# Layer norm's statistics moved within the layer, weight pieces worked two steps later, and the second MLP's tokens loaded one layer earlier, in a three-stage kernel

## The reference

```
kv = k^T v per head;  out = q kv;  out = out / rms(out) * g_norm
x  = out as (batch, token, 512)
u  = x + real(fft2(x));  un = layernorm(u)
x2 = u + relu(un @ w_ch1) @ w_ch2            (512 -> 2048 -> 512)
u2 = x2 + (x2^T @ U @ V)^T                   (tokens mixed, rank 32)
out = u2 + relu(u2 @ w2_ch1) @ w2_ch2
```

## Time and profile before

| | |
|---|---|
| median of 3 runs | 1805.35 us (1803.37 to 1811.79) |
| the profiled execution: its own time | 1805.91 us |
| its span, first to last instruction | 1804.1 us |
| granted TensorE clock, mean | 0.985 of full speed |
| busy share of the span: PE, DVE, ACT, POOL | 95%, 77%, 44%, 20% |
| DMA: moved, mean | 478.53 MB, 265 GB/s |

### The profile page before, as it was taken

One profiled execution on the slowest core, in us unless ns is written; L12 is line 12 of the kernel. 1 busy time (PEld: TensorE's weight loads), 2 busy tenths in 40 slices (PEclk: granted clock), 3 DMA queues, 4 the chain that ended last, 5 costly groups with the idle time before them and its releaser, 6 DMA issues.

```text
span 1804.1 us, 27550 instructions
## 1 busy us (share of the span) xinstructions
PE 1721.0 (95%) x10772; PEld 1659.3 (92%) x10772; DVE 1381.1 (77%) x1679; ACT 784.9 (44%) x1126; POOL 364.4 (20%) x308
## 2 busy tenths in 40 slices
PE   6789979989999999999999999999999999999999
PEld 5667769979998999999999999999999999999999
DVE  4779986997797788887876866956947757758567
ACT  2333334644554554554444445435434434443443
POOL 2889974231010010010010021010100100100200
PEclk9899989999999999999999999999999999999999
DMA  7477557998788798898887777866766756767663
GB/s 259 152 269 248 198 199 273 338 346 323 285 331 305 288 342 304 298 344 305 310 311 240 251 251 256 320 231 238 252 234 246 266 210 252 252 222 260 230 243 128
DMA packets 124977, 478.53 MB, mean 265 GB/s; under 512 B 12401, under 2 KB 49777, under 8 KB 84146
## 3 DMA queue, kind: packets, MB, share of 16 engines
q1 hardware_dynamic: 123634, 475.60, 74.3%
q10 hardware_dynamic: 1216, 1.18, 0.2%
HBM read 398.09 MB, written 78.64 MB: 264 GB/s over the span
## 4 chain that ended last, share of the span: by engine, by line
PE 75%; DVE 14%; DMA 3%; issue 3%; POOL 3%; ACT 1%; SPq 1%; DVEq 0%; POOLq 0%; ACTq 0%
PE pair L869 11%; PE pair L871 10%; PE pair L870 10%; PE pair L900 6%; PE pair L901 6%; PE pair L902 6%; PE pair L889 5%; PE pair L892 5%; PE pair L891 5%; DVE t_lo L1406 3%; PE pair L672 2%; DMA in_sb<-x_dram 1%; DVE t_raw L1425 1%; PE tr_ps L765 1%; DVE w_sb L1338 1%
## 5 line engine op out<-in xcount | busy, mean ns | idle before, releaser
L869 PE MATMUL pair<-t_hi,w_sb 128*128 128x384 f32 x1344 | 459.9, 342 | 10.1 <-DVE h_sb L1443 8.3
L870 PE MATMUL pair<-t_lo,w_sb 128*128 128x384 f32 x1344 | 455.7, 339 | 0.0
L871 PE MATMUL pair<-t_hi,w_sb 128*128 128x384 f32 x1344 | 455.6, 339 | 0.0
L1643 POOL TENSOR_TENSOR t_raw<-a_sb 128x768 f32<-128x768 f32 x60 | 127.2, 2124 | 1206.9 <-PE pair L892 476.1
L1116 ACT ACTIVATE t_hi<-t_raw 128x768 fp32r<-128x768 f32 x240 | 202.6, 847 | 278.9 <-DVE t_raw L1425 278.9
L1406 DVE TENSOR_TENSOR t_lo<-t_raw,t_hi 128x768 fp32r<-128x768 f32 x300 | 306.4, 1026 | 9.5 <-ACT t_hi L1104 8.2
L889 PE MATMUL pair<-w_sb,t_hi 128*128 128x256 f32 x1008 | 285.4, 283 | 8.0 <-DVE t_lo L1406 8.0
L891 PE MATMUL pair<-w_sb,t_hi 128*128 128x256 f32 x1008 | 283.5, 281 | 0.0
L892 PE MATMUL pair<-w_sb,t_lo 128*128 128x256 f32 x1008 | 283.5, 281 | 0.0
L869 PEld LDWEIGHTS pair<-t_hi,w_sb 128*128 128x128 f32 x1344 | 252.6, 188 | 17.6 <-issue 12.4
L870 PEld LDWEIGHTS pair<-t_lo,w_sb 128*128 128x128 f32 x1344 | 252.8, 188 | 3.0
(11 more groups left out here) (158 smaller groups left out, 2370.5 us busy)
## 6 DMA issues: line engine op xcount, KB each, us to landing
w_sb<-wc SPq DMA_DIRECT2D x268, 1024.0 KB, 5.2
wc<-w_sb SPq DMA_DIRECT2D x20, 1024.0 KB, 6.5
w_raw<-wr1a SPq DMA_DIRECT2D x24, 512.0 KB, 5.7
w_raw<-wr1b SPq DMA_DIRECT2D x24, 512.0 KB, 4.1
wc<-pb SPq DMA_DIRECT2D x16, 640.0 KB, 4.8
w_raw<-wr2a SPq DMA_DIRECT2D x10, 1024.0 KB, 7.3
wc<-pb_v SPq DMA_DIRECT2D x16, 640.0 KB, 5.4
q_sb<-q_t SPq DMA_DIRECT2D x8, 1152.0 KB, 9.3
```

The lines of the kernel that those rows point to most:

```text
L869: nc.tensor.matmul(ps, w_hi, hi[:, x, :], start=(fresh and x == 0), stop=False, skip_group_check=True)
L870: nc.tensor.matmul(ps, w_hi, lo[:, x, :], start=False, stop=False, skip_group_check=True)
L871: last = nc.tensor.matmul(ps, w_lo, hi[:, x, :], start=False, stop=(x == 1), skip_group_check=True)
```

## The change

`LN_AT` goes from 14, 17, 26 to 8, 13, 26, so statistics stand at 8, 13, 26 and the normalising at 10, 15, 28. `load_in` at steps 2 and 4 stays for the layers up to 6; the first four chunks of layers 7 to 11 (normed or mixed, and turned, one layer before the products use them) are asked for at steps 44 and 46 of the layer before that, g = 5 to 9, instead of steps 2 and 4 of g = 6 to 10. Unit and job: the sum from t+4 to t+6, ACT's split from t+7 to t+8, DVE's from t+8 to t+9, the store from t+8 to t+10.

```diff
--- before.py
+++ after.py
@@ -149,7 +149,7 @@
 
 OUT_AT = [1 + 3 * j for j in range(NCH)]
 GATHER_AT = [4 + 3 * j for j in range(NCH)]
-LN_AT = [14, 17, 26]
+LN_AT = [8, 13, 26]
 
 
 def mix_at(g):
@@ -633,21 +633,25 @@
                         store_u(B - 1)
 
                     if g < NG - 1:
-                        if t in (2, 4):
+                        if t in (2, 4) and g + 1 <= NS:
                             load_in(NCH * (g + 1) + t - 2)
                             load_in(NCH * (g + 1) + t - 1)
+
+                        if t in (44, 46) and NS < g + 2 < NG:
+                            load_in(NCH * (g + 2) + t - 44)
+                            load_in(NCH * (g + 2) + t - 43)
                         if t in in_load_at(g):
                             load_in(NCH * (g + 1) + 4 + in_load_at(g).index(t))
 
                     if (g, t) in UNIT_AT:
                         load_unit(UNIT_AT[g, t])
-                    if (g, t - 8) in UNIT_AT:
-                        store_unit(UNIT_AT[g, t - 8])
+                    if (g, t - 10) in UNIT_AT:
+                        store_unit(UNIT_AT[g, t - 10])
 
                     if (g, t) in JOB_AT:
                         load_job(JOB_AT[g, t])
-                    if (g, t - 8) in JOB_AT:
-                        store_job(JOB_AT[g, t - 8])
+                    if (g, t - 10) in JOB_AT:
+                        store_job(JOB_AT[g, t - 10])
                     n = NSLOT * g + j
                     if n + 3 in RAW_SLOTS and stored_slot(n + 3):
                         store_w(n + 3)
@@ -1229,10 +1233,10 @@
                             take_in(NCH * (g + 1) + in_at(g).index(t - 1))
                         if g + 1 < NS and t - 1 in LN_AT:
                             deviation(3 * (g + 1) + LN_AT.index(t - 1))
-                    if (g, t - 7) in UNIT_AT:
-                        split_unit_hi(UNIT_AT[g, t - 7])
-                    if (g, t - 7) in JOB_AT:
-                        split_job_hi(JOB_AT[g, t - 7])
+                    if (g, t - 8) in UNIT_AT:
+                        split_unit_hi(UNIT_AT[g, t - 8])
+                    if (g, t - 8) in JOB_AT:
+                        split_job_hi(JOB_AT[g, t - 8])
                     for n in RAW_SLOTS:
                         if NSTEP * g + t == max(0, 2 * n - 7):
                             split_slot_hi(n)
@@ -1577,14 +1581,14 @@
                                 layer_norm(3 * (g + 1) + LN_AT.index(t - 2))
                         elif t - 1 in mix_at(g):
                             add_mixed(NCH * (g + 1) + mix_at(g).index(t - 1))
-                    if (g, t - 4) in UNIT_AT:
-                        sum_unit(UNIT_AT[g, t - 4])
-                    if (g, t - 4) in JOB_AT:
-                        sum_job(JOB_AT[g, t - 4])
-                    if (g, t - 8) in UNIT_AT:
-                        split_unit_lo(UNIT_AT[g, t - 8])
-                    if (g, t - 8) in JOB_AT:
-                        split_job_lo(JOB_AT[g, t - 8])
+                    if (g, t - 6) in UNIT_AT:
+                        sum_unit(UNIT_AT[g, t - 6])
+                    if (g, t - 6) in JOB_AT:
+                        sum_job(JOB_AT[g, t - 6])
+                    if (g, t - 9) in UNIT_AT:
+                        split_unit_lo(UNIT_AT[g, t - 9])
+                    if (g, t - 9) in JOB_AT:
+                        split_job_lo(JOB_AT[g, t - 9])
                     for n in RAW_SLOTS:
                         if NSTEP * g + t == max(0, 2 * n - 6):
                             split_slot_lo(n)
```

## The result

The changed kernel takes 1797.4 us (median of 10 runs, 1792.65 to 1801.31) against 1806.3 us (10 runs, 1801.99 to 1812.91): a ratio of 0.995, 95% interval 0.9931 to 0.9969. The forecast was 1795.2 us. The profiled execution has a span of 1796.1 us against 1804.1, 8.0 us less. Every ratio in this document is against executions of the kernel before that were taken alongside, and leaves out three slow ones: 1826.2 us of the kernel before (experiments 1 to 4), and 2359.5 and 2110.9 us of the 11 in experiment 6.

The account below looks back on a forecast made before the run. PE, busy 1721.0 of 1804.1 us, was taken to bound the kernel, its waits all ending with late DVE results. The sum was 1805.91 - 18.1 (parts 1 and 2) + 7.2 + 0.2 = 1795.2 us, range 1786.5 to 1804.5.

Parts of the forecast that it names:

- Part 1, tokens a layer ahead: Layers 7 to 10: PE's waits on the first mixed chunk vanish, gain 7.6 us; layer 7's own move brings nothing.
- Part 2, what leaves steps 6, 14 and 17: Waits after step 7 (4.4 us) and at step 19 (5.3 us in layers 1 to 4, 0.8 in layer 0) vanish.
- Part 3, what comes late: Layers 1 to 4: new PE waits at four places, 1.8 us a layer, 7.2 in four; layer 0 loses 0.2.
- step 13: Layers 1 to 4: `x_lo` for the gather after this step late by 0.6 us, its slot's low part held by POOL.
- step 16: Layers 1 to 4: gather late by 0.5 us, as step 15's normalising stands before m7 and `x_lo`.
- step 24: Layers 1 to 4: late by 0.3 us, as the job's sum moves to 22, ahead of m5.
- step 42: Down half of layers 1 to 4: operand late by 0.4 us, as the unit's sum and low part move later.
- The port: Steps 8 to 13: the unit's low part starts at 11.64, ahead of POOL (about 12.3); POOL runs 13.1 to 14.95.
- The loss of 0.2 us at step 12: Layer 0: DVE waits at step 8 for late first chunks, so step 12's operand comes at 291.4, due at 291.3.
- The step that failed: Second splits at 52 and 53, ACT's one-step move and stores at t+10 cost nothing; stores land in some 6 us.
- case "forecast": Whole kernel: gains and new waits as counted, 1795.2 us; chance 0.50, of which 0.31 beyond the 0.5% line.
- only part 1 is left: Rival: several small waits (gathers, m5) return the whole gain of layers 0 to 4, 1798.3 us; chance 0.11.

Follow-up runs that it names:

- experiment 1: Kernel before, with only the token loads of layers 7 to 11 moved a layer ahead: ratio 0.9959 to the kernel before, median 1797.4 us.
- experiment 2: Kernel before, with only layer norm's statistics moved to steps 8 and 13: ratio 0.9982 (0.9957 to 1.0007) to the kernel before.
- experiment 3: Kernel before, with only the weight pieces (units and jobs) moved later: ratio 1.0013 (0.999 to 1.0037) to the kernel before.
- experiment 4: Changed kernel, with layer 5's zeroing of `vp_raw` moved from step 0 to 4, its loads and splits four steps later: ratio 0.995 to the kernel before.
- experiment 6: Changed kernel, with the jobs and the down half's units back as before, only up-half units late: ratio 0.9931 to the kernel before.
- experiment 7: Changed kernel, with 1.2 us more DVE work before the unit's low part in layers 1 to 4: 1399.4 us from layer 1 to the end, one execution.
- experiment 10: Changed kernel, with jobs and down-half units back as before and the second normalising at step 14, not 15: 1788.7 us, ratio 0.992 to the kernel before.
- experiment 9: Changed kernel, with only the jobs' stores back at t+8, ahead of the slot's weight load: ratio 0.9957 (0.9943 to 0.9971) to the kernel before.
- experiment 5: Changed kernel, with the jobs back at t+4, t+7, t+8, t+8 and the units left late: ratio 0.9957 (0.9934 to 0.998) to the kernel before.
- experiment 8: Changed kernel run again unaltered, for a second profile: ratio 0.9967 (0.9947 to 0.9988) to the kernel before.

## Why the prediction was right, and where it was not

- *What bounds the kernel.* "All end with DVE" overlooked one wait of layer 0, on ACT:

```profile
PE pair L869 <- ACT h_sb L1133: 1.8, 1, 1.8
```

After the change it was 0.5 us; no edit aims at it.
- *Part 1, tokens a layer ahead, 7.6 us.* Right: 7.6 in layers 7 to 10, and 7.6 when done alone. The chunk's wait on DVE is gone, and layer 7's move brought nothing.
- *Part 2, what leaves steps 6, 14 and 17.* Right in place. The waits at 7 and 19 are gone in every profile that has the edit, and each edit alone removes its own. The 0.2 us a wait added to the idle time held: in layer 4 step 7 is 0.43 us shorter where 0.22 stood as idle, and the step before 19 1.36 shorter where 1.1 stood.
- *Part 3, what comes late.* All four places are right. Sizes by step lengths, forecast against measured: step 13 0.6 against 0.3 to 0.4, step 16 0.5 against 0.5, step 24 0.3 against 0.4, step 42 0.4 against 0.4; in sum 1.8 against 1.6 to 1.7 us a layer. Only the chain to step 13 was over-sized: DVE was 0.3 us earlier than counted, by tenths from the sum on, and POOL's sum, forecast to end at 14.95, ended at 14.7. That layers 1 to 4 came out at -2.3 where -2.5 was forecast is in part luck: the new waits were about 0.6 us smaller in sum, and the slower pace of three down halves (last section) gave 1.0 us back.
- *The port.* By the trace the forecast's order holds in the changed kernel, and experiment 7 made the other order. The Trainium skill ("SBUF — State Buffer", "🔬 SBUF: two separate sides") says that whoever starts first has the shared pair for the whole instruction and the other one waits. Both orders agree with it: with DVE first POOL's sum lasted 2.12 to 2.41 us and not 1.84, with POOL first DVE's low part lasted 2.77 and not 1.48.
- *Layer 0.* DVE waited for the chunk at step 8, 1.06 us where some 2 were forecast, for it was still busy with a late low part before; m7 was forecast to be delayed by 2.4 us. In the profile after, m7 begins at 288.97, 2.1 us after the place it had before (19.3 us into the layer, now 21.5). The loss of 0.2 us at step 12 did not come: step 11 took 2.12 us as before. Of the 4.3 us by which the layer is shorter the edit explains under one. Layer 0 took 139.8 and 137.4 us in experiments 1 and 3, which leave layer norm as it was, and 140.8 and 141.6 in experiments 2 and 4, which move it: it varies by 4 us whatever the edit, and the profile's 4.3 us is mostly that. A good part is the clock: after PE's wait for step 24 (2.38 us before, 2.19 after) that step took 4.10 us at a fallen clock in the kernel before and 2.55 in the changed one. It is slow in five of the twelve profiles; in experiments 3 and 10 it followed a wait of the same 2.38 us and was not.
- *The step that failed* is the one that priced the stores at nothing: "ACT's move by one step and the stores at t+10 cost nothing", because SP "has its store landed (some 6 us, as the loads) before the load four steps (8.5 us) on". I asked who waits for the store on SP's queue and found the next load into the same buffer. I did not ask who else waits for it: DVE's zeroing of `vp_raw`, at step 0 of layer 5. Nor did I see that t+10 puts the store behind the slot's weight load and not before it, which brings its landing from 5.5 to 9.3 us. It cost 3.9 us with the clock's fall (2.1 and 3.0 in the profiles without it). The half of that step that I had looked at held: in the changed kernel SP waited for stores before the next loads, 5.5 us in sum and 1.8 at the longest, and none of PE's waits came from there. The profile's 8.0 us came near the forecast's 10.7 although a term was missing, because layer 0's luck was of its size; from layer 1 to the end the forecast was 10.1 us less and the measured difference 5.4. By the medians the gain is 8.9 us, 1.8 short of the forecast, and the interval (0.9931 to 0.9969, that is 5.6 to 12.5 us less) holds both.
- *The chances.* The result lies at the edge that was drawn at 0.5%. By its waits the case "forecast" is the one that happened, with one wait more. By its number the rival "only part 1 is left" (1798.3 us) fits as well: the tokens alone give a median of 1797.4 us, as the whole change does. What parts 2 and 3 won in layers 1 to 4 was returned, though not by the several small waits of that rival but by the one store in layer 5 and the slower pace. Experiments 6, 9 and 10 take part of it back.

## What to carry to other kernels

When a step is moved later, list every wait on the semaphores it raises, in all engines and in the next stage too, not only the wait that guards the same buffer; the last instance of a repeated piece is where such a wait bites. In a queue that issues transfers, compare what stands directly ahead of the moved one: half a microsecond later but behind a 1 MB load was 4 to 5 us later at the landing here. Where two engines hold a port against each other, count which of them starts first: 0.4 us of order decided over 1.3 us of length here. And run each part of a change alone: here the first part had the whole gain, and the other two together won nothing on top as long as the last store came late.

## What the runs showed that I had not expected

- A 1 MB store landed in 4.8 us ahead of a 1 MB load and in 9.3 to 10.0 us behind it, issued at the same moment of the step (experiment 9, the changed kernel twice; the last of eight stores, and the other seven agree).
- In layers 1 to 5 the granted clock fell to 1.2 GHz after PE waits of 2.15 us (changed kernel, layer 5), 2.36 us (experiment 7, layer 5) and 2.89 us (experiment 5, layer 1). It did not after 2.8 us in the same place of the same kernel (experiment 8), after 2.20 us (kernel before, layer 2), nor after the four of 2.22 to 2.51 us of experiment 7. So the length of one wait does not tell, and the runs do not settle what does.
- In the down halves of layers 1 to 4 the steps have more than one pace, whatever the kernel: 2.115 us in all four layers of the kernel before, some 0.024 us more in each step from the 33rd on in all four layers of experiment 1 and in two of experiment 6, and 2.16 us from step 43 on in layer 2 of experiment 5, with no wait shown. The slower pace makes 0.5 us a layer, as much as one of the waits argued about here. The runs don't show what sets it; three of the four layers of the changed kernel's profile have it from step 43 on (60.9 us, of which 0.4 is step 42's wait). A pace also moves a wait: where the slower one ran up to step 41 (experiment 8, layers 1 to 4), that step took 2.29 us instead of 2.41.
- The edits do not add up as edits of their own. Layer norm alone made a wait at step 12 that the whole change doesn't have (experiment 2), and the jobs put back alone made one at step 55 (experiment 5).
